# Two linked expert layers in Strassen form on one core: the order of the first pair's products, the opening's loads, the last step and GpSimd's pacing are changed

## Chip, cores and metric

The kernel runs on one core of one Trainium2 chip. The metric is the device time of one execution in microseconds (us), the median over the runs shown.

## What is computed

All inputs and the output are float32.

```python
# attention in chunks of 64 tokens: B, H, S, D = 8, 8, 576, 64
attn = softmax(q_c @ k_c.T / sqrt(D)); out = attn @ v_c
x = out as [4608, 512]
h = x @ w_in1                       # [512, 2048]
x = (max(h, 0) + alpha * min(h, 0)) @ w_out1     # [2048, 512]
h = x @ w_in2
y = (h - tanh(h)) @ w_out2          # [4608, 512]
```

## The kernel before

**Numbers.** Each float32 operand of a large product is split into a high part (a copy rounded to fp32r) and a low part (the operand less its high part). A product is then hi*hi + hi*lo + lo*hi, three matmuls.

**Supertiles and phases.** The 4608 tokens are cut into 6 supertiles of 768, and each layer goes over them once, so there are 12 supertiles, s = 0 to 11 (0 to 5 are layer 0, 6 to 11 are layer 1). Each has a phase A (the product with w_in) and a phase B (the product with w_out). Supertiles 0 and 1 do phase B in 32 plain units; from s = 2 on it is done in 28 steps of two blocks each.

**Phase A** takes the 2 x 2 blocks of x and of the weights by Strassen's scheme (Winograd's form): 8 pairs p of slices of the hidden dimension, 7 products P1 to P7 for each, so 56 products. A product is 6 matmuls of 384 columns, reads one weight block and adds into a PSUM bank. P1 and P2 share a bank, P6, P7 and P4 another, P5 and P3 a third. Between them ScalarE copies P1 to `s1` (`copy_s1`, line 925), VectorE makes u2 = s1 + bank after P6 (`sum_u2`, line 1252) and u3 = s1 + bank after P7 (`sum_u3`, line 1258). P2 waits for `s1_ready`. P7 adds into the bank that u2 is read from, and so waits for `u2_ready` (in `product`, i == 7); P4 waits for `u3_ready`. The order of the products is written out twice: as the places of their weight blocks (`product_at`) and as TensorE's calls in `phase_a` of `block.tensor`. For the first pair it is P1(0), P1(1), P5(0), P6(0), P2(0), P7(0), P6(1), P4(0); later pairs go P6, P1, P4 of the pair before, P5, P3 of the pair before, P2, P7.

**Phase B.** For each unit or step ScalarE makes the high part of g (`high_g`, line 981), VectorE the low part (`low_g`, line 1306), and TensorE waits for it (`glo_ready`). VectorE also makes Strassen's sums (`g_sum`, line 1328) and the activation (lines 1284 and 1300). In layer 1 a step's block is 9 matmuls of 256 columns over three tiles m of 128 tokens (lines 768 to 770). After the last block of the last supertile VectorE adds 768 columns to the stage (`read_y12`, line 1352) and the SyncE queue stores them (`store_quarter`, line 1610).

**Weight blocks.** A ring in SBUF holds 4 groups of 4 blocks. In supertile 0 the blocks are made in place: ScalarE writes the high part (`high_part`, 868), GpSimd the sums (`weight_sums`, 484 to 490) and the low part (`low_part`, 495). From supertile 1 on the SyncE queue loads whole groups of 1 MB from DRAM (`load_group`, 1593), three groups ahead, each when the group four before it has been used. The 168 blocks of steps and of layer 1 are made beside the other work by GpSimd, in the order of the list `MADE`: `keep_block` waits until TensorE has reached the block that `pace(k)` names, casts (510), subtracts (512) and stores 256 KB (515), with three places in turn. `pace` is a table of (supertile, count, first block, spacing in tenths of a block). `load_group` waits for the stores of the blocks in its group at s = 2 from group 14 on and at s = 6 (`made_stored`, 1592). If GpSimd falls behind the table, its blocks follow one another without pause.

**The opening.** 6 units of attention come first. SyncE's queue issues the loads of q and k, v and the raw weights in a written order. TensorE does scores (609), transposes (616) and outputs (633) of the units; VectorE subtracts the maximum and normalizes (1165 to 1189); ScalarE takes exponents (879) and copies (900, 908). Then come the splits of x (919, 1218) and its differences T1 to T4 (1214). `bank_free` holds each P1, P5 and P6 of supertile 0 until all 6 units are copied (`x_copied`).

## Time and profile before

| | us |
|---|---|
| three runs | 1540.65, 1540.56, 1536.16 |
| their median | 1540.56 |
| the profiled execution | 1540.17 |
| its span, first to last instruction | 1538.4 |
| TensorE busy in the span | 1508.9 (98%) |
| VectorE busy | 1202.3 (78%) |
| ScalarE busy | 723.7 (47%) |
| GpSimd busy | 574.3 (37%) |

The rows of the trace give a start in us from the start of the span, a duration in us, the engine (PE is TensorE, DVE is VectorE, ACT is ScalarE, POOL is GpSimd, SPq is SyncE's queue), the line of the kernel and the tiles written and read. A bracket gives the idle time of the engine before the row and what ended it. TensorE's matmuls overlap: each is issued while the one before it still runs, so what counts is the distance from start to start, and the duration of a row is longer.

### The profile page before, as it was taken

Reading aid. Unit: us, or ns where it says so; the run is one execution under the profiler, and the core shown is the slowest. Engines: PE = TensorE matmul, PEld = TensorE weight load, DVE = VectorE, ACT = ScalarE, POOL = GpSimd, SP = SyncE. Lnnn points to the kernel's source line nnn. Section 1 sums busy time; section 2 is a strip of 40 time slices with the busy share of each in tenths; the row PEclk is TensorE's granted clock in tenths of the full one; section 3 lists DMA queues with packets and bytes.
Section 4 is the critical chain, followed back from the end, with each engine's and each line's share of the span. In section 5 each row is a group of like instructions: output and inputs, shape, how many; then the busy total and the mean of one; then the engine's idle time right before and its main releaser. Section 6 shows DMA issues by size and latency. Waiting matters only on the chain.

```text
span 1538.4 us, 30313 instructions
## 1 busy us (share of the span) xinstructions
PE 1508.9 (98%) x11622; PEld 1487.0 (97%) x11622; DVE 1202.3 (78%) x1555; ACT 723.7 (47%) x1379; POOL 574.3 (37%) x756
## 2 busy tenths in 40 slices
PE   6999999999999999999999999999999999999998
PEld 5999999999999999999899999999999999999998
DVE  7998678869969987996796796786686686687684
ACT  5566465546546546652353343343344344244243
POOL 3973367877547547646736750000000000000000
PEclk8999999999999999999999999999999999999999
DMA  7795897799999899999989989768768768867765
GB/s 261 265 317 199 337 358 277 262 353 359 323 350 376 308 360 369 337 301 376 356 288 374 355 315 319 283 247 290 290 245 287 297 246 282 300 248 267 272 246 179
DMA packets 105341, 464.41 MB, mean 302 GB/s; under 512 B 12528, under 2 KB 35056, under 8 KB 62960
## 3 DMA queue, kind: packets, MB, share of 16 engines
q1 hardware_dynamic: 87344, 404.27, 73.5%
q0 software_dynamic: 17568, 57.69, 9.7%
q8 instruction: 95, 1.56, 0.4%
q10 hardware_dynamic: 288, 0.52, 0.1%
q14 instruction: 46, 0.38, 0.1%
HBM read 376.45 MB, written 85.98 MB: 301 GB/s over the span
## 4 chain that ended last, share of the span: by engine, by line
PE 84%; DVE 9%; issue 3%; DMA 2%; ACT 1%; POOL 1%; SPq 0%; DVEq 0%; ACTq 0%
PE banks L689 14%; PE banks L691 14%; PE banks L690 13%; PE banks L768 7%; PE banks L770 7%; PE banks L769 7%; PE banks L761 4%; PE banks L762 4%; PE banks L763 4%; DVE go_lo L1306 3%; PE banks L718 3%; PE banks L719 3%; PE banks L720 3%; DVE g_full L1328 2%; DVE g_full L1284 1%
## 5 line engine op out<-in xcount | busy, mean ns | idle before, releaser
L689 PE MATMUL banks<-xo_hi,ring 128*128 128x384 f32 x1344 | 454.6, 338 | 2.9 <-DMA ring<-w_split 1.4
L691 PE MATMUL banks<-xo_hi,ring 128*128 128x384 f32 x1344 | 450.2, 335 | 0.0
L690 PE MATMUL banks<-xo_lo,ring 128*128 128x384 f32 x1344 | 449.9, 335 | 0.0
L1306 DVE TENSOR_TENSOR go_lo<-g_full,go_hi 128x768 fp32r<-128x768 f32 x344 | 352.3, 1026 | 68.7 <-ACT go_hi L981 66.1
L981 ACT CAST go_hi<-g_full 128x768 fp32r<-128x768 f32 x344 | 286.1, 837 | 252.7 <-PE banks L770 101.5
L768 PE MATMUL banks<-ring,go_hi 128*128 128x256 f32 x1008 | 285.7, 283 | 0.5 <-issue 0.2
L769 PE MATMUL banks<-ring,go_hi 128*128 128x256 f32 x1008 | 285.2, 283 | 0.0
L770 PE MATMUL banks<-ring,go_lo 128*128 128x256 f32 x1008 | 285.2, 283 | 0.0
L689 PEld LDWEIGHTS banks<-xo_hi,ring 128*128 128x128 f32 x1344 | 253.0, 188 | 7.1 <-issue 2.6
L691 PEld LDWEIGHTS banks<-xo_hi,ring 128*128 128x128 f32 x1344 | 252.9, 188 | 0.4 <-issue 0.4
L690 PEld LDWEIGHTS banks<-xo_lo,ring 128*128 128x128 f32 x1344 | 253.1, 188 | 0.0
L768 PEld LDWEIGHTS banks<-ring,go_hi 128*128 128x128 f32 x1008 | 193.3, 192 | 1.0 <-issue 1.0
L769 PEld LDWEIGHTS banks<-ring,go_hi 128*128 128x128 f32 x1008 | 193.4, 192 | 0.0
L770 PEld LDWEIGHTS banks<-ring,go_lo 128*128 128x128 f32 x1008 | 193.4, 192 | 0.0
L1328 DVE TENSOR_TENSOR g_full<-g_full 128x768 f32<-128x768 f32 x160 | 166.9, 1043 | 0.0
L761 PE MATMUL banks<-go_hi,ring 128*128 128x384 f32 x448 | 150.7, 336 | 6.1 <-DVE go_lo L1306 3.1
L762 PE MATMUL banks<-go_lo,ring 128*128 128x384 f32 x448 | 149.8, 334 | 0.0
L763 PE MATMUL banks<-go_hi,ring 128*128 128x384 f32 x448 | 149.8, 334 | 0.0
L925 ACT COPY s<-banks 128x384 f32<-128x384 f32 x96 | 45.9, 479 | 173.1 <-PE banks L691 172.8
L510 POOL CAST sums<-raw 128x256 fp32r<-128x256 f32 x112 | 77.0, 687 | 132.0 <-issue 81.9
L1258 DVE TENSOR_TENSOR u<-s,banks 128x384 f32<-128x384 f32 x96 | 53.0, 552 | 91.6 <-PE banks L691 91.5
L1284 DVE SCALAR_TENSOR_TENSOR g_full<-stage,alpha_rest,g_full 128x768 f32<-128x768 f32 (+1 forms) x102 | 119.5, 1213 | 3.7 <-ACT stage L952 3.7
(138 smaller groups left out, 2346.5 us busy)
## 6 DMA issues: line engine op xcount, KB each, us to landing
ring<-w_split SPq DMA_DIRECT2D x302, 1024.0 KB, 7.1
w_split<-sums POOLq DMA_DIRECT2D x112, 256.0 KB, 6.7
w_split<-ring SPq DMA_DIRECT2D x22, 1024.0 KB, 5.5
qkv<-in_chunks SPq DMA_DIRECT2D x60, 256.0 KB, 6.9
w_split<-made_first POOLq DMA_DIRECT2D x56, 256.0 KB, 6.8
raw<-in_weights POOLq DMA_DIRECT2D x48, 256.0 KB, 7.5
x_raw<-y_between SPq DMA_DIRECT2D x6, 1536.0 KB, 10.5
out<-stage SPq DMA_DIRECT2D x24, 384.0 KB, 8.3
```

What stands on the lines that cost most here:

```text
L689: nc.tensor.matmul(h, hi, xo_hi[:, o, k, :], start=fresh and k == 0, stop=False, skip_group_check=not fresh)
L690: nc.tensor.matmul(h, hi, xo_lo[:, o, k, :], start=False, stop=False, skip_group_check=not fresh)
L691: last = nc.tensor.matmul(h, lo, xo_hi[:, o, k, :], start=False, stop=k == 1, skip_group_check=not fresh)
L761: nc.tensor.matmul(y, hi, go_hi[:, slot, e, :], start=begin, stop=False, skip_group_check=not fresh)
L762: nc.tensor.matmul(y, hi, go_lo[:, slot, e, :], start=False, stop=False, skip_group_check=not fresh)
L763: last = nc.tensor.matmul(y, lo, go_hi[:, slot, e, :], start=False, stop=end, skip_group_check=not fresh)
L768: nc.tensor.matmul(y, hi, w[:, 0, :], start=begin and m != 1, stop=False, skip_group_check=not fresh or m == 1)
L769: nc.tensor.matmul(y, hi, w[:, 1, :], start=False, stop=False, skip_group_check=not fresh or m == 1)
L770: last = nc.tensor.matmul(y, lo, w[:, 0, :], start=False, stop=end, skip_group_check=not fresh or m == 1)
L981: nc.scalar.copy(go_hi[:, go_slot(s, n), :, :], g_of(s, n)).then_inc(ghi_ready, 1)
L1306: nc.vector.tensor_tensor(go_lo[:, slot, :, :], g_of(s, n), go_hi[:, slot, :, :], ALU.subtract).then_inc(glo_ready, 1)
L1328: nc.vector.tensor_tensor(g_pairs(q, to), g_pairs(q, a), g_pairs(q, b), ALU.subtract).then_inc(t_ready, 1)
```

## The change

It has four parts. The first pair's order becomes P1(0), P1(1), P2(0), P5(0), P6(0), P7(0), in `product_at` and in TensorE's calls. In the opening the raw weights' loads move behind later loads of q, k and v, P1 and the second pair's P5 and P6 wait for 3 and 4 copied units in place of 6, and ScalarE's calls are put in another order. The last step of the last supertile does tiles 0 and 1 of both blocks first and tile 2 after them, with the sum and the store in two pieces. The table of `pace` gives 41, 17, 29, 29, 25 and 27 blocks to supertiles 1 to 6 in place of 44, 20, 27, 27, 25 and 25. The loop in `load_group` is rewritten for a group in which one of the three places has no block.

```diff
--- before.py
+++ after.py
@@ -71,7 +71,7 @@
     if i == 3:
         return base(p + 1) + 4 if p < PAIRS - 1 else 55
     if p == 0:
-        return {1: 0, 5: 2, 6: 3, 2: 4, 7: 5}[i]
+        return {1: 0, 2: 2, 5: 3, 6: 4, 7: 5}[i]
     if p == 1 and i in (1, 6):
         return 1 if i == 1 else base(1) + 1
     return base(p) + {6: 0, 1: 1, 5: 3, 2: 5, 7: 6}[i]
@@ -177,8 +177,8 @@
 
 def pace(k):
 
-    for s, count, first, tenths in ((1, 18, 2, 30), (1, 26, FIRST_BLOCKS, 12), (2, 17, 2, 26), (2, 3, 76, 110), (3, 20, 2, 26), (3, 7, 60, 70),
-                                    (4, 20, 2, 26), (4, 7, 60, 70), (5, 19, 2, 22), (5, 6, 72, 70), (6, 17, 2, 22), (6, 8, 57, 20)):
+    for s, count, first, tenths in ((1, 16, 2, 30), (1, 25, FIRST_BLOCKS, 12), (2, 15, 2, 28), (2, 2, 76, 150), (3, 21, 2, 26), (3, 8, 60, 60),
+                                    (4, 21, 2, 25), (4, 8, 60, 60), (5, 19, 2, 24), (5, 6, 72, 60), (6, 19, 2, 22), (6, 8, 57, 20)):
         if k < count:
             return s, first + tenths * k // 10
         k -= count
@@ -274,6 +274,7 @@
         ghi_ready, glo_ready = sem("ghi_ready"), sem("glo_ready")
         y_even_read, y_odd_read = sem("y_even_read"), sem("y_odd_read")
         g_first_ready, t_ready, p1_copied = sem("g_first_ready"), sem("t_ready"), sem("p1_copied")
+        last_front = sem("last_front")
         u2_copied, u3_copied = sem("u2_copied"), sem("u3_copied")
         y11_ready, y12_ready, y21_ready, y22_ready = sem("y11_ready"), sem("y12_ready"), sem("y21_ready"), sem("y22_ready")
 
@@ -640,7 +641,8 @@
                 if p >= 2:
                     pe.wait_ge({1: c11_read, 5: c12_ready, 6: c21_ready}[i], after_pairs(s, p - 2))
                 elif s == 0:
-                    pe.wait_ge(x_copied, UPS)
+
+                    pe.wait_ge(x_copied, 3 if i == 1 else 4 if p else UPS)
                 elif plain(s - 1):
                     if i == 1:
                         if p == 0:
@@ -770,6 +772,26 @@
                             last = nc.tensor.matmul(y, lo, w[:, 0, :], start=False, stop=end, skip_group_check=not fresh or m == 1)
                     last.then_inc(block_done, 1)
 
+            def last_step(s, n):
+
+                i, slot = STEPS[n][0], go_slot(s, n)
+                for e in range(2):
+                    weights_ready(s, step_at(n, e))
+                pe.wait_ge(glo_ready, go_count(s, n))
+                for tiles in ((0, 1), (2,)):
+                    for e in range(2):
+                        w = block_of(s, step_at(n, e))
+                        for m in tiles:
+                            hi, lo = go_hi[:, slot, e, m * P:(m + 1) * P], go_lo[:, slot, e, m * P:(m + 1) * P]
+                            y = banks[:, bank_pair(i) + m // 2, m % 2 * 256:(m % 2 + 1) * 256]
+                            nc.tensor.matmul(y, hi, w[:, 0, :], start=False, stop=False, skip_group_check=True)
+                            nc.tensor.matmul(y, hi, w[:, 1, :], start=False, stop=False, skip_group_check=True)
+                            last = nc.tensor.matmul(y, lo, w[:, 0, :], start=False, stop=e == 1, skip_group_check=True)
+                        if m == 2:
+                            last.then_inc(block_done, 1)
+                    if m == 1:
+                        last.then_inc(last_front, 1)
+
             def attention(s, n):
                 for u in range(UPS):
                     age = unit_age(s, u, n)
@@ -783,9 +805,9 @@
             def phase_a(s):
                 product(s, 1, 0)
                 product(s, 1, 1)
+                product(s, 2, 0)
                 product(s, 5, 0)
                 product(s, 6, 0)
-                product(s, 2, 0)
                 product(s, 7, 0)
                 product(s, 6, 1)
                 product(s, 4, 0)
@@ -824,8 +846,12 @@
                     product(s, 4, PAIRS - 1)
                     step(s, 0, (1,))
                     product(s, 3, PAIRS - 1)
-                    for n in range(1, len(STEPS)):
+                    for n in range(1, len(STEPS) - 1):
                         step(s, n)
+                    if s < RUNS - 1:
+                        step(s, len(STEPS) - 1)
+                    else:
+                        last_step(s, len(STEPS) - 1)
 
             pe.wait_ge(ident_ready, 1)
             scores(0)
@@ -1113,9 +1139,9 @@
                 nc.scalar.dma_start(here[:, 1, :], there[:, 1, :]).then_inc(qk_first_in[u], 16)
             exponent(0)
             exponent(1)
-            high_parts(0, 0)
             place_attnT(0)
             exponent(2)
+            high_parts(0, 0)
             copy_x(0)
             high_parts(0, 2)
             place_attnT(1)
@@ -1131,12 +1157,12 @@
             high_parts(0, 8)
             copy_x(3)
             high_x(0, B11)
+            place_attnT(4)
             high_x(0, B21)
-            place_attnT(4)
+            place_attnT(5)
             high_parts(0, 10)
-            place_attnT(5)
+            copy_x(4)
             high_parts(0, 11)
-            copy_x(4)
             copy_x(5)
             high_x(0, T1)
             copy_s1(0, 0)
@@ -1347,8 +1373,15 @@
 
             def read_y12(s):
 
+                dve.wait_ge(u2_copied, once(s))
+                if s == RUNS - 1:
+                    to = y_quarter(s, 0, 1)
+                    dve.wait_ge(last_front, 1)
+                    nc.vector.tensor_tensor(to[:, 0:512], to[:, 0:512], banks[:, bank_pair(3), :], ALU.add).then_inc(y12_ready, 1)
+                    dve.wait_ge(block_done, block_base(s) + blocks_of(s))
+                    nc.vector.tensor_tensor(to[:, 512:], to[:, 512:], banks[:, bank_pair(3) + 1, 0:256], ALU.add).then_inc(y12_ready, 1)
+                    return
                 dve.wait_ge(block_done, block_base(s) + blocks_of(s))
-                dve.wait_ge(u2_copied, once(s))
                 nc.vector.tensor_tensor(y_quarter(s, 0, 1), y_quarter(s, 0, 1), sum_banks(s, 3), ALU.add).then_inc(y12_ready, 1)
 
             def attention(s, n):
@@ -1587,9 +1620,9 @@
                     sp.wait_ge(w_stored[q % RING], 16 * stores_of(q))
                 if s == PLAIN and q >= 14 or s == SUPER:
                     for i in range(3):
-                        last = max(k for k in range(i, len(MADE), 3)
-                                   if MADE[k][0] == layer_of(s) and MADE[k][1] // PER_GROUP <= q)
-                        sp.wait_ge(made_stored[i], 16 * (last // 3 + 1))
+                        here = [k for k in range(i, len(MADE), 3) if MADE[k][0] == layer_of(s) and MADE[k][1] // PER_GROUP <= q]
+                        if here:
+                            sp.wait_ge(made_stored[i], 16 * (here[-1] // 3 + 1))
                 sp.dma_start(ring[:, group % RING, :, :, :].rearrange("x b h n -> x (b h n)").bitcast(F32),
                              w_dram[dram_group(layer_of(s), q, plain(s)), :, :]).then_inc(ring_in[group % RING], 16)
 
@@ -1673,12 +1706,12 @@
             load_first_qk(0)
             load_first_qk(1)
             load_first_v(0)
-            load_raw(0)
             load_first_qk(2)
             load_first_v(1)
-            load_raw(1)
+            load_raw(0)
             load_first_qk(3)
             load_first_v(2)
+            load_raw(1)
             load_first_qk(4)
             load_first_v(3)
             load_first_qk(5)
@@ -1692,9 +1725,13 @@
                     make_groups(s)
                 else:
                     load_groups(s)
-            store_quarter(RUNS - 1, 0, 1)
+            for count, tiles in ((0, 2), (1, 1)):
+                sp.wait_ge(y12_ready, once(RUNS - 1) + count)
+                here = stage[:, 2 * HALF + 512 * count:2 * HALF + 512 * count + 256 * tiles]
+                sp.dma_start(out_tiles[SUPER - 1, 3 + 2 * count:3 + 2 * count + tiles, :, 0:256].rearrange("j p d -> p j d"),
+                             here.rearrange("x (j d) -> x j d", j=tiles)).then_inc(y_stored[0], 16)
             for half in range(2):
-                sp.wait_ge(y_stored[half], 16 * y_stores(RUNS - 1))
+                sp.wait_ge(y_stored[half], 16 * (y_stores(RUNS - 1) + (half == 0)))
             for i in range(RING):
                 sp.wait_ge(w_stored[i], 16 * sum(1 for g in range(i, group_base(1), RING)))
```

## Rows read from the trace of the kernel before

**Rows 1.** First line of the page.

```profile
span 1538.4 us, 30313 instructions
```

**Rows 2.** Engines' busy time by stretch: start of phase B, s = 2; phases B, s = 5, 7.

```profile
378.00:398.00 20.00, 18.27 (x101) 17.18 (x101) 19.60 (x20) 8.69 (x12) 17.58 (x22) 1.00 0.94 314
...
757.00:820.00 63.00, 60.61 (x349) 60.03 (x348) 60.87 (x61) 31.40 (x40) 32.28 (x40) 1.00 0.88 300
...
996.00:1058.00 62.00, 62.00 (x513) 62.00 (x512) 51.83 (x59) 31.63 (x41) 0.00 (x0) 1.00 0.72 257
```

**Rows 3.** Timeline of TensorE, s = 9: last matmul of P6(0), first of P7(0).

```profile
1181.69 0.33 PE L691 MATMUL banks<-xo_hi,ring 128*128 128x384 f32 x1
...
1182.91 0.34 PE L689 MATMUL banks<-xo_hi,ring 128*128 128x384 f32 x1
```

**Rows 4.** Timelines of VectorE and ScalarE, s = 9: u2 of pair 0, copy of P1(0).

```profile
1182.12 0.55 DVE L1252 TENSOR_TENSOR u<-s,banks 128x384 f32<-128x384 f32 x1 [3.27 <-PE banks L691]
...
1178.94 0.48 ACT L925 COPY s<-banks 128x384 f32<-128x384 f32 x1 [6.63 <-PE banks L691]
```

**Rows 5.** Timelines where TensorE waited for VectorE, s = 2, step 2.

```profile
384.38 1.15 DVE L1306 TENSOR_TENSOR go_lo<-g_full,go_hi 128x768 fp32r<-128x768 f32 x1
...
385.67 0.41 PE L761 MATMUL banks<-go_hi,ring 128*128 128x384 f32 x1 [0.74 <-DVE go_lo L1306]
385.92 0.34 PE L762 MATMUL banks<-go_lo,ring 128*128 128x384 f32 x1
```

**Rows 6.** Timeline of the opening and of the first products.

```profile
2.13 1.07 SPq L1570 DMA_DIRECT2D raw<-in_weights  x2
...
10.32 1.05 DVE L1189 TENSOR_TENSOR probs<-probs,row_inv 128x512 f32<-128x512 f32 x1
...
10.65 1.14 PE L609 MATMUL banks<-g_full 64*64 64x64 f32 x32 [3.72 <-DMA g_full<-in_chunks]
...
11.85 0.69 DVE L1165 TENSOR_REDUCE row_max<-banks 128x8 f32<-128x512 f32 x1 [0.48 <-PE banks L609]
...
31.30 0.58 ACT L908 COPY x_raw<-banks 128x512 f32<-128x512 f32 x1 [0.35 <-PE banks L633]
...
31.98 0.66 PE L689 MATMUL banks<-xo_hi,ring 128*128 128x384 f32 x1 [0.75 <-issue]
...
38.69 0.54 DVE L1252 TENSOR_TENSOR u<-s,banks 128x384 f32<-128x384 f32 x1
...
39.33 0.41 PE L689 MATMUL banks<-xo_hi,ring 128*128 128x384 f32 x1
```

**Rows 7.** Timeline of the end: VectorE's last sum.

```profile
1534.40 0.95 DVE L1352 TENSOR_TENSOR stage<-stage,banks 128x768 f32<-128x768 f32 x1 [4.59 <-PE banks L770]
```

**Rows 8.** Timeline of GpSimd, s = 2: its first idle time.

```profile
405.80 4.15 POOL L510 CAST sums<-raw 128x256 fp32r<-128x256 f32 x1 [7.36 <-issue]
```

**Rows 9.** Groups of VectorE by line, s = 2: 384 to 398, then 404 to 441 us.

```profile
L1306 DVE TENSOR_TENSOR go_lo<-g_full,go_hi 128x768 fp32r<-128x768 f32 x6 | 8.1, 1358 | 0.0
...
L1306 DVE TENSOR_TENSOR go_lo<-g_full,go_hi 128x768 fp32r<-128x768 f32 x17 | 16.8, 986 | 2.2 <-ACT go_hi L981 2.0
```

**Rows 10.** Timelines of GpSimd's stores, SyncE's ring loads and TensorE in s = 6.

```profile
866.17 0.56 POOL L515 DMA_DIRECT2D w_split<-sums  x1 [0.30 <-POOL sums L512]
...
873.01 0.56 POOL L515 DMA_DIRECT2D w_split<-made_first  x1 [0.30 <-POOL made_first L512]
...
875.44 0.80 SPq L1593 DMA_DIRECT2D ring<-w_split  x2
...
882.66 0.28 PE L768 MATMUL banks<-ring,go_hi 128*128 128x256 f32 x1
...
913.36 0.56 POOL L515 DMA_DIRECT2D w_split<-sums  x1 [0.30 <-POOL sums L512]
...
918.88 0.80 SPq L1593 DMA_DIRECT2D ring<-w_split  x2
```

**Rows 11.** DMA issues, 875.0 to 875.8 us: count, KB, us to landing.

```profile
ring<-w_split SPq DMA_DIRECT2D x1, 1024.0 KB, 4.8
```

## Prediction

> **What bounds the kernel now.** I read the busy times first, then TensorE's row of starts block by block, and at each gap the row of the engine that ended it. TensorE is the bound nearly everywhere. In phase B of s = 7 it is busy 62.00 of 62.00 us, and the same holds from s = 7 to the end; only earlier is there something to save: 1.73 us idle in the first 20 us of phase B of s = 2, 2.39 us in phase B of s = 5 [rows 2]. There VectorE is the one that is late (19.60 of 20 us and 60.87 of 63 us busy), while GpSimd works beside it. So the reader should ask of each part: does it put a wait into a stream of matmuls that has none, and which of the few early waits does it take out?
>
> **P2 third.** No product is added or removed. What moves is the cover between P6(0) and P7(0). P7(0) adds into the bank that u2 is made from, so it needs P6(0) finished, then VectorE's sum, then the signal. Before, P2(0) ran in that time. At s = 9 the last matmul of P6(0) starts at 1181.69 and P7(0) at 1182.91: seven starts later, so one start is (1182.91 - 1181.69) / 7 = 0.174 us, and six of these are P2(0) [rows 3]. VectorE's sum starts at 1182.12 and takes 0.55, so it ends 0.98 us after P6(0)'s last start [rows 4]. From such an end to TensorE's first matmul: 384.38 + 1.15 = 385.53, and the matmul starts at 385.67, 0.14 us later [rows 5]. The chain is 0.98 + 0.14 = 1.12 us and the cover was 1.22 us: hidden, by 0.1 us. After the change P7(0) comes right behind P6(0); the cover is 0.174 us, and 1.12 - 0.17 = 0.95 us is a wait. The matmul that starts after a wait holds its successor back too: 385.92 - 385.67 = 0.25 us in place of 0.174 [rows 5], 0.07 us more. Each first pair costs **1.0 us**. The bounds are 0.9 (signal 0.1 us, no hold) and 1.05.
>
> What does P2 third give back? P2(0) needs the copy of P1(0), which ends at 1178.94 + 0.48 = 1179.42 [rows 4]; it would start twelve starts ahead of 1181.69 + 0.17, at 1179.78, so it doesn't wait, but with only 0.3 us to spare. P5(0) and P6(0) come one product later, and in supertiles 1 to 11 they had no wait to lose. Behind the waiting P7(0) stand P6(1), P4(0) and the rest of TensorE's queue; VectorE's u3 waits for P7(0) and moves with it. VectorE had stood idle 3.27 us before u2 [rows 4], so it can't use the 1.0 us to catch up either; its later work hangs on products that are late by as much. I therefore count all of supertiles 1 to 11: 11 x 1.0 = **+11.0 us** (9.9 to 11.5).
>
> In supertile 0 the wait is there already: u2 starts at 38.69, after VectorE's splits of x, and P7(0) at 39.33 [rows 6]. No charge there.
>
> **The opening.** Unit 2's scores start at 10.65, on the load of q and k; VectorE goes on at 11.85, after 0.48 us of idle time [rows 6]. The load now takes the place of two raw loads that held the queue from 2.13 for 1.07 us, so it is issued 1.1 us sooner. VectorE can then go on when its normalization ends, 10.32 + 1.05 = 11.37: 0.48 us gained. That normalization ran beside GpSimd's weight sums, which now start later; it might be shorter, but the same GpSimd work then meets a later normalization. From 11.85 to unit 5's output VectorE and the units follow one another, so the gain arrives. P1(0) starts at 31.98, after the copy of unit 5, 31.30 + 0.58 [rows 6]; it no longer waits for it, 0.7 us sooner. But u2 and P7(0) hang on T1 to T3, which still need that copy, so what lasts is the shift of the copy. I take **-0.7** (nothing to -1.5). A raw load now lands later, and the casts behind it on ScalarE stand ahead of unit 1's copy: up to 0.3 us back, inside this range.
>
> **The last step.** The last sum takes 0.95 us for 768 columns [rows 7]; 384 columns take 0.55 [rows 4], so 256 take about 0.95 - 512 x (0.40 / 384) = 0.42: -0.53 us. The first piece, about 0.7 us long, can start six matmuls before the end and just fits. The second store is a third as large, and the first is still in flight in the same queue: nothing to -0.5. I take **-0.6** (-0.3 to -1.0). TensorE does the same 18 matmuls. The rewritten loop in the ring's loads names the same stores: nothing.
>
> **GpSimd's table.** Through s = 1 and 2 GpSimd is behind its table (in s = 2 by over 20 us), so it works without pause, and only the number of its blocks counts, some 3.4 us each ((873.01 - 866.17) / 2 [rows 10]). Before, the run is 43 blocks long and ends at 398.4, where its first idle time begins (405.80 - 7.36 [rows 8]); now it has 40 from the same start, so it ends three blocks, 10 us, sooner, near 388. In 384 to 398 us VectorE's low parts take 1.36 us on average, in 404 to 441 us 0.99 [rows 9]: nine such operations and more get 0.4 us shorter. The idle time at 385.67 stays, most of what follows it goes: **-1.6** of some 2.6 us (0 to -2.6). The Trainium skill (SBUF — State Buffer, section "Who interferes with whom") says that VectorE and GpSimd share a port pair as an exclusive lock, the loser blocked for the other's whole instruction. By that rule even more is freed here, the full -2.6, and the sum below would be 1550; the rows show an operation stretched by 0.4 us on average, and I go by them. The blocks taken out here reappear: one more in phase A and one in phase B of s = 3 and 4, two more in s = 6. I charge +0.5, +0.3 and +0.4 us of VectorE's waits (0 to 1 us each).
>
> **The ring in s = 6.** Here the change meets a limit. GpSimd is behind its table in s = 6 as well, and group 15 of the ring needs made block 154. That was stored from 866.17, and SyncE's queue could issue only at 875.44, though TensorE had left the ring's place 12 blocks of 1.04 us before 882.66, at 870.2 [rows 10]. The load took 4.8 us [rows 11], so it landed at 880.3; TensorE needs the group at 882.66 [rows 10]: 2.4 us to spare. Now two blocks stand ahead, and block 154 is stored where block 156 was, at 873.01 [rows 10]: 6.8 us later. TensorE is 1.0 us later. If the store takes as long as before (9.3 us to the queue's release) the group lands at 882.3 + 4.8 = 887.1, 3.4 us late; if it takes the 5.5 us of the last block (913.36 to 918.88 [rows 10]) it lands at 883.4 and is just in time. The second is nearer, as the DMA queues are idle while SyncE waits. The last made block is the same case again: issued 913.36 + 7, released at 926, landed at 931, needed near 929 with the delays. Together **+1.5** (0 to +6).
>
> **Sum.** Against the profiled execution, 1540.17 us (a span of 1538.4 [rows 1] and 1.8 us around it), 0.4 us below the median of the runs: +11.0 - 0.7 - 0.6 - 1.6 + 0.5 + 0.3 + 0.4 + 1.5 = +10.8, so 1551.0 us.
>
> **Rivals.**
> 1. **The late ring decides** in s = 6: both groups at their upper bound, +6 and more in place of +1.5. 1540.2 + 15.3 = 1555.5 or above. For it: the queue already waited 5 us there twice. Against: the store is fast when nothing else loads. 0.12.
> 2. **The waits are absorbed** in supertiles 1 to 6, where TensorE waits later for VectorE anyway: 1.0 us there is worth nothing. Left are 5 x 1.0 in s = 7 to 11 and the rest of the sum: 1545. Against: VectorE is idle before u2. 0.10.
> 3. **Faster:** the early waits all go. From s = 1 to s = 6 TensorE's waits for VectorE and for loads come to some 12.8 us; if fewer blocks of GpSimd, and a pause of TensorE in which the engines and queues ahead catch up, remove them all, the sum is +11.0 - 0.7 - 0.6 - 12.8 = -3.1, 1537 us. It decides from 9.7 us removed. Against: s = 3, 4 and 6 get more blocks, not fewer. 0.04.
> 4. **No wait at P7(0):** only if P7 did not need u2; `product` says it does. That the change doesn't do what it says I give 0.01, near 1538.5.
>
> The forecast has 0.73. What a measurement of this kernel can tell is about 0.3%, 4.6 us: slower means above 1545.2. The forecast and the first rival are slower, the second lies on the line. Faster 0.04, same 0.08, slower 0.88. The forecast's own range is 1547 to 1554; with half of the first two rivals, 1545.5 to 1556.5.
>
> **What would show it.** At each first P7 of s = 1 to 11 TensorE's row should show a wait of 0.9 us, released by VectorE's line of u2, also in s = 7 to 11, where TensorE is now never idle. GpSimd's run in s = 2 should end 10 us earlier, and the gaps behind step 4 be gone. SyncE's queue should stand before groups 15 and 25 in s = 6. I am wrong if P7(0) starts 0.17 us behind P6(0), or if the later gaps of s = 2 to 6 shrink by what the first pairs lose.

## The result and the profile after

The changed kernel takes 1547.83 us (median of 5 runs, 1546.71 to 1550.94), beside 1540.56 for the kernel before (5 runs, 1536.16 to 1542.66). The two medians lie 7.3 us apart. The ratio on record, with its 95% interval, is 1.0057 [1.0042, 1.0073], which is 8.8 us, between 6.5 and 11.2: slower, clear of noise. The forecast was 1551.0, with a range from 1545.5 to 1556.5. The profiled execution took 1546.71 us.

The first place to look is TensorE's row where P7(0) follows P6(0). The next three fences are timelines of the kernel after at s = 9: TensorE, VectorE, and ScalarE with the copy of P1(0). They answer to [rows 3] and [rows 4].

```profile
1187.30 0.34 PE L693 MATMUL banks<-xo_hi,ring 128*128 128x384 f32 x1
1188.39 0.41 PE L691 MATMUL banks<-xo_hi,ring 128*128 128x384 f32 x1 [0.75 <-issue]
1188.64 0.34 PE L692 MATMUL banks<-xo_lo,ring 128*128 128x384 f32 x1
```

```profile
1187.73 0.55 DVE L1278 TENSOR_TENSOR u<-s,banks 128x384 f32<-128x384 f32 x1 [4.24 <-PE banks L693]
```

```profile
1183.51 0.48 ACT L951 COPY s<-banks 128x384 f32<-128x384 f32 x1 [6.63 <-PE banks L693]
```

The last matmul of P6(0) starts at 1187.30 and P7(0) at 1188.39, 1.09 us later, where one start takes 0.174. That is 0.916 us of waiting. (The bracket says 0.75, since it counts from the end of the matmul before.) The next matmul comes 0.25 us after it, another 0.075. So the first pair loses 0.99 us, and it does so in each of s = 1 to 11. VectorE's u2 ends at 1187.73 + 0.55 = 1188.28, and P7 starts 0.11 us behind it. The copy of P1(0) ends at 1183.51 + 0.48 = 1183.99, and P2(0) starts at 1184.35 without a wait: 0.36 us to spare, as reckoned.

In the list of what TensorE waited for, in the kernel after, these waits stand under "issue" and not under VectorE (columns: us in all, times, longest). They are the first line here. The second line is P7(0) of supertile 0. Before, the same line of the kernel had one wait under "issue", that of P1(0) of supertile 0, and none at any P7(0) of s = 1 to 11.

```profile
PE banks L691 <- issue: 8.2, 11, 0.8
...
PE banks L691 <- DVE u L1278: 1.4, 1, 1.4
```

The reader should not stop at the word "issue": it is what the profile writes where it saw no releaser at the moment of the start. Here the sum had ended 0.11 us earlier, and only the two timelines side by side show the cause.

The busy time by stretch of the kernel after answers to [rows 2]: the first 20 us of phase B of s = 2, and then phases B of s = 3 to 7.

```profile
378.00:398.00 20.00, 20.00 (x118) 20.00 (x117) 18.80 (x25) 10.47 (x14) 3.09 (x6) 1.00 0.88 315
506.30:570.00 63.70, 61.11 (x350) 60.21 (x349) 61.78 (x62) 31.81 (x42) 34.20 (x41) 1.00 0.93 333
637.80:702.00 64.20, 61.47 (x349) 60.05 (x349) 62.82 (x62) 32.14 (x42) 32.78 (x40) 1.00 0.91 310
759.20:822.00 62.80, 61.56 (x349) 60.05 (x349) 59.80 (x62) 32.15 (x42) 29.23 (x35) 1.00 0.87 313
879.20:942.60 63.40, 62.89 (x518) 62.69 (x518) 59.17 (x59) 31.79 (x41) 31.85 (x39) 1.00 0.88 328
999.80:1062.40 62.60, 62.60 (x518) 62.60 (x518) 51.82 (x59) 31.43 (x40) 0.00 (x0) 1.00 0.73 258
```

In s = 2 TensorE has no idle time left in these 20 us; GpSimd works 3.09 us there in place of 17.58. In s = 3 and 4 GpSimd's column has grown, and VectorE's with it. The same two phases in the kernel before:

```profile
508.50:570.90 62.40, 61.06 (x351) 60.34 (x350) 58.72 (x61) 31.85 (x41) 26.99 (x34) 1.00 0.91 328
637.50:698.80 61.30, 60.79 (x349) 60.21 (x349) 59.14 (x62) 32.56 (x42) 24.96 (x32) 1.00 0.89 307
```

At s = 4 GpSimd goes from 32 to 40 instructions and VectorE from 59.14 of 61.30 us to 62.82 of 64.20. What TensorE waited for in that stretch was one wait of 0.4 us before, and after it is this:

```profile
PE banks L763 <- DVE go_lo L1332: 1.5, 2, 1.3
PE banks L763 <- issue: 1.2, 1, 1.2
```

In phase B of s = 3 TensorE's longest wait is not for VectorE but for a weight group of the ring. The kernel before has none there:

```profile
PE banks L763 <- DMA ring<-w_split: 1.0, 1, 1.0
```

I cut each span at the starts of the stages' first matmuls. The last two columns are means over the profiled executions of the kernels of this study with the old table and without the wait (five), and with the new table and the wait (three):

| us | before | after | mean, old table, no wait | mean, new table, wait |
|---|---|---|---|---|
| up to phase B of s = 0 | 92.83 | 92.28 | | |
| phases A, s = 1 to 6 | 383.30 | 385.67 | 383.87 | 386.20 |
| phases B, s = 2 to 6 | 314.14 | 314.67 | 312.74 | 315.36 |
| phases A, s = 7 to 11 | 280.89 | 285.80 | 280.91 | 285.77 |
| last matmul's start to the end | 4.29 | 3.31 | | |

Phases A of s = 7 to 11 pay the full price, 4.9 us for five waits. Phases A of s = 1 to 6 pay 2.4 us for six (2.3 by the means). The opening and the tail give 0.55 and 0.98 us back, phase B of s = 0 takes 0.32, and with phases B of s = 2 to 6 it makes the span's 1544.9 - 1538.4 = 6.5 us.

The opening in the kernel after, in answer to [rows 6]: unit 2's scores, the normalization, GpSimd's first sum of weights, VectorE going on, the first product, the copy of unit 5.

```profile
8.21 1.13 PE L610 MATMUL banks<-g_full 64*64 64x64 f32 x32 [1.38 <-DMA g_full<-in_chunks]
...
9.76 0.69 DVE L1215 TENSOR_TENSOR probs<-probs,row_inv 128x512 f32<-128x512 f32 x1
...
10.27 0.76 POOL L485 TENSOR_TENSOR sums<-raw 128x256 f32<-128x256 f32 x1 [8.80 <-DMA raw<-in_weights]
...
10.37 0.68 DVE L1191 TENSOR_REDUCE row_max<-banks 128x8 f32<-128x512 f32 x1
...
30.62 0.69 PE L691 MATMUL banks<-xo_hi,ring 128*128 128x384 f32 x1
...
30.75 0.59 ACT L934 COPY x_raw<-banks 128x512 f32<-128x512 f32 x1
```

VectorE goes on at 10.37 in place of 11.85. The load is earlier, so there is no idle time, and the normalization takes 0.69 in place of 1.05 us: GpSimd's first sum now starts at 10.27, near its end, and no longer stands beside all of it. Of these 1.48 us the copy of unit 5 keeps 0.55.

The end in the kernel after, in answer to [rows 7]:

```profile
1541.28 0.69 DVE L1380 TENSOR_TENSOR stage<-stage,banks 128x512 f32<-128x512 f32 x1 [3.95 <-PE banks L789]
...
1541.61 0.28 PE L789 MATMUL banks<-ring,go_lo 128*128 128x256 f32 x1
...
1541.92 0.42 DVE L1382 TENSOR_TENSOR stage<-stage,banks 128x256 f32<-128x256 f32 x1
```

The first piece of the sum runs under the last matmuls, and the second takes 0.42 us as reckoned. The last store of the output landed 2.1 us after its issue in place of 2.6.

The ring in s = 6, in answer to [rows 10]: the stored block that group 15 needs, and SyncE's load; then TensorE's first matmul on the group, and its first on group 16. Ahead of them, GpSimd's first pause in s = 2, in answer to [rows 8].

```profile
402.27 1.01 POOL L511 CAST sums<-raw 128x256 fp32r<-128x256 f32 x1 [20.80 <-issue]
...
872.91 0.56 POOL L516 DMA_DIRECT2D w_split<-sums  x1 [0.30 <-POOL sums L513]
...
879.96 6.25 SPq L1626 DMA_DIRECT2D ring<-w_split  x4
...
885.70 0.28 PE L770 MATMUL banks<-ring,go_hi 128*128 128x256 f32 x1
...
890.69 0.39 PE L770 MATMUL banks<-ring,go_hi 128*128 128x256 f32 x1 [0.51 <-DMA ring<-w_split]
```

```profile
ring<-w_split SPq DMA_DIRECT2D x1, 1024.0 KB, 5.2
```

Block 154 is stored from 872.91, 0.1 us from the forecast's 873.01. The load of 5.2 us lands at 885.2 and TensorE takes it at 885.70, without a wait: 0.5 us to spare. The next load was held up in the queue too: it was issued 0.5 us behind the first, took 10.2 us and landed at 890.6, and there TensorE waited 0.51 us. In the second profile of the changed kernel that load took 9.4 us and landed 0.4 us ahead of its use. Group 25 landed at 927.9, 1.7 us ahead of its use.

### The profile page after: what moved, and what is told of

Read it like the earlier page. It is cut to its first block, busy times and chain, and to the rows that moved or that the text cites. A ratio compares the mean times of both kernels' runs of the same rounds, so it can differ in the third digit from the quotient of the medians.

```text
span 1544.9 us, 30314 instructions
## 1 busy us (share of the span) xinstructions
PE 1510.2 (98%) x11622; PEld 1485.0 (96%) x11622; DVE 1208.1 (78%) x1556; ACT 723.8 (47%) x1379; POOL 566.1 (37%) x756
## 4 chain that ended last, share of the span: by engine, by line
PE 87%; DVE 6%; issue 3%; DMA 2%; POOL 1%; ACT 1%; SPq 0%; DVEq 0%; ACTq 0%; POOLq 0%
PE banks L691 14%; PE banks L692 14%; PE banks L693 14%; PE banks L770 8%; PE banks L772 8%; PE banks L771 8%; PE banks L763 4%; PE banks L764 4%; PE banks L765 4%; PE banks L720 3%; PE banks L721 3%; PE banks L722 3%; DVE go_lo L1332 2%; DMA ring<-w_split 1%; DVE g_full L1310 1%
## 5 line engine op out<-in xcount | busy, mean ns | idle before, releaser
L513 POOL TENSOR_TENSOR sums<-raw,sums 128x256 fp32r<-128x256 f32 x112 | 116.0, 1036 | 9.2
```

## The experiments

Eleven runs on three chips. Each median stands beside that of the kernel before on the same chip (1539.92, 1539.48 and 1539.50), except the first, which is a single execution. Where two kernels ran on different chips, their ratios to the kernel before are the better comparison. All were profiled once. The diffs show the lines that carry each edit, and `...` stands for what is left out.

**The kernel before, once more.**

> The kernel before, unchanged, profiled once more, to see how much TensorE's waits vary between two executions. If the waits before late loads (1.95 us before an output of unit 16 in s = 1, 1.58 us in the middle of phase A of s = 5) belong to the order of the work, both stand again within 0.5 us; if they are chance of the DMA queues, one or both are gone. The waits for VectorE in s = 2 to 6 should stand again within 0.3 us each. P7(0) has no wait in s = 1 to 11 by either theory.

1537.52 us, span 1535.7. TensorE's waits for loads in phase A of s = 1 differ between the two executions of the same kernel. Before, and then again:

```profile
PE a_bank L633 <- DMA qkv<-in_chunks: 1.6, 2, 1.0
```

```profile
PE a_bank L633 <- DMA qkv<-in_chunks: 1.1, 1, 1.1
```

Phase B of s = 5 took 63.25 and 61.41 us, so the waits for VectorE there did not stand again within the 0.3 us that was expected. One profile carries about 2 us of such chance, so stages are compared by means over several kernels below.

**P2 third alone.** The new order on the kernel before, and the rewritten loop of `load_group`, which names the same stores. Everything else is old.

```diff
-        return {1: 0, 5: 2, 6: 3, 2: 4, 7: 5}[i]
+        return {1: 0, 2: 2, 5: 3, 6: 4, 7: 5}[i]
...
+                product(s, 2, 0)
                 product(s, 5, 0)
                 product(s, 6, 0)
-                product(s, 2, 0)
                 product(s, 7, 0)
```

> The kernel before with P2 of the first pair third, and nothing else. Theory (the cover between P6(0) and P7(0) is gone): TensorE waits 0.91 us at P7(0) in each of s = 1 to 11, each supertile loses 0.99 us, 10.9 us in all, 1551 us; the other waits stay. Rival (waits are absorbed by later ones where VectorE is late): 0.99 us in s = 7 to 11 alone, 5 us in all, and the waits of s = 2 to 6 in phase B shrink by as much. Rival (the slowdown is the ring's or the table's): no more than 1 us slower.

1549.58 against 1539.92: 1.0058 [1.0044, 1.0072], +9.7 us by the medians, 6.8 to 11.1 by the interval. TensorE's waits:

```profile
PE banks L689 <- issue: 9.0, 12, 0.8
```

This one edit costs all that the whole change costs. Eleven of the twelve waits are P7(0) of s = 1 to 11; the twelfth is P1(0) of s = 0, which the kernel before has too. P7(0) of s = 0 waits as well, filed under GpSimd. There the fourth product starts 0.8 us later than before, and that is the granted clock: from 36 to 38 us it is 0.55 of full speed here, near the lower level of 1.2 GHz, and 0.98 in the kernel before (second line).

```profile
36.00:38.00 2.00, 2.00 (x8) 2.00 (x8) 2.00 (x3) 1.47 (x3) 1.38 (x2) 0.55 0.01 4
```

```profile
36.00:38.00 2.00, 2.00 (x13) 2.00 (x12) 2.00 (x3) 1.47 (x3) 1.44 (x2) 0.98 0.01 4
```

**P2 back in the fifth place, the rest of the change kept.**

```diff
-        return {1: 0, 2: 2, 5: 3, 6: 4, 7: 5}[i]
+        return {1: 0, 5: 2, 6: 3, 2: 4, 7: 5}[i]
...
-                product(s, 2, 0)
                 product(s, 5, 0)
                 product(s, 6, 0)
+                product(s, 2, 0)
                 product(s, 7, 0)
```

> The changed kernel with the old order of the first pair (P1, P1, P5, P6, P2, P7). Theory: 10.9 us faster than the changed kernel in s = 1 to 11, up to 1 us given back in the opening, as P5(0) again needs T1 as the third product: 1537 to 1538 us, faster than before by 3 to 4 us. Rival (table and ring cause the slowdown): 1546 us or more, no faster than the changed kernel.

1539.38: 0.9997 [0.9987, 1.0008]. Against the changed kernel that is 8.4 us less, and against the kernel before nothing: the 3 to 4 us that were expected below it are not there.

**P2 third, but P5 and P6 exchanged,** so that P5(0) stands between P6(0) and P7(0).

```diff
-        return {1: 0, 2: 2, 5: 3, 6: 4, 7: 5}[i]
+        return {1: 0, 2: 2, 6: 3, 5: 4, 7: 5}[i]
...
                 product(s, 2, 0)
-                product(s, 5, 0)
                 product(s, 6, 0)
+                product(s, 5, 0)
                 product(s, 7, 0)
```

> The changed kernel with P5(0) and P6(0) exchanged, so that P5(0) runs while VectorE makes u2: P1, P1, P2, P6, P5, P7. The work is the same. Theory (only the missing cover costs): the 0.91 us wait at P7(0) is gone in s = 1 to 11 though P2 is still third, 10.9 us less than the changed kernel, 1537 us, 0.2% below before. Rival (P2 third costs in another way, by the place of its block in the ring or the earlier copy of P1): the time stays near 1547 us. If P6(0) now waits for T2 in the opening, that wait is there in place of the one at P7(0), and P7(0) starts when it did.

1539.81: 0.9999 [0.9988, 1.0010], 8.0 us less than the changed kernel, though not the 1537 that was expected. TensorE and then VectorE at s = 9; the first row is the end of P6(0), the second the last matmul of P5(0), the third P7(0):

```profile
1180.48 0.33 PE L693 MATMUL banks<-xo_hi,ring 128*128 128x384 f32 x1
...
1181.52 0.34 PE L693 MATMUL banks<-xo_hi,ring 128*128 128x384 f32 x1
1181.70 0.34 PE L691 MATMUL banks<-xo_hi,ring 128*128 128x384 f32 x1
```

```profile
1180.91 0.56 DVE L1278 TENSOR_TENSOR u<-s,banks 128x384 f32<-128x384 f32 x1 [3.20 <-PE banks L693]
```

u2 ends at 1181.47 and P7 starts at 1181.70, 0.174 behind the matmul ahead of it. P2 is third here too. So its early place costs nothing by itself; what costs is that nothing stands between P6 and P7.

**The new table alone.**

```diff
-    for s, count, first, tenths in ((1, 18, 2, 30), (1, 26, FIRST_BLOCKS, 12), (2, 17, 2, 26), (2, 3, 76, 110), (3, 20, 2, 26), (3, 7, 60, 70),
+    for s, count, first, tenths in ((1, 16, 2, 30), (1, 25, FIRST_BLOCKS, 12), (2, 15, 2, 28), (2, 2, 76, 150), (3, 21, 2, 26), (3, 8, 60, 60),
...
```

> The kernel before with the new table of GpSimd's blocks, and nothing else. From the profile of the changed kernel: TensorE's idle time in phase B of s = 2 falls by 2.5 to 3 us, in s = 3 and 4 it rises by 1.4 and 2 to 3 us, s = 6 doesn't change; no difference in sum, 1539 to 1542 us. Rival: the rise in s = 3 and 4 came from the shifted first pair, and the table alone saves 3 us, 1537 us. SyncE's queue stands before groups 15 and 25 of s = 6 longer than before, but TensorE waits there under 1 us.

1540.98 against 1539.48: 1.0007 [0.9997, 1.0018]. Its phases B of s = 2 and s = 4:

```profile
378.40:438.90 60.50, 60.50 (x350) 60.33 (x349) 54.62 (x62) 32.54 (x42) 9.04 (x12) 1.00 0.89 318
...
637.80:701.00 63.20, 61.46 (x349) 60.11 (x348) 61.63 (x61) 31.79 (x41) 30.47 (x37) 1.00 0.91 308
```

The waits of s = 2 are all gone, 2.9 us less than the 63.39 of the kernel before. But s = 4 takes 63.25 in place of 61.35. Means of six kernels with each table, phases B of s = 2 to 6: 63.00, 62.35, 61.34, 62.76, 63.29 with the old one, and 60.69, 63.25, 63.56, 64.26, 63.82 with the new one. That is -2.3, +0.9, +2.2, +1.5 and +0.5, together +2.8 us. Two things stand beside these means. In s = 3 five of the six kernels with the new table wait 0.3 to 1.0 us for a group of the ring near 553 us, and none with the old one does. In s = 4 the changed kernel takes 64.25 and 64.21 in its two profiles and the other four 63.21 to 63.25, and why it takes 1 us more is open.

**The opening alone.**

```diff
-            load_raw(0)
             load_first_qk(2)
             load_first_v(1)
-            load_raw(1)
+            load_raw(0)
...
```

> The kernel before with the opening's loads, ScalarE's order and the shorter waits of P1, P5 and P6 in supertile 0 alone; P2 stays fifth. Forecast of the text: VectorE's chain to unit 5 is 0.5 to 1.3 us shorter, and phase B of supertile 0 starts 0.5 us earlier or more, since P7(0) hangs on VectorE's splits of x. If P2 third had its own part in that, phase B starts no earlier than before (92.8 us in the first profile, 93.2 in the second).

1539.50: 1.0002 [0.9990, 1.0013]. Phase B of s = 0 begins at 92.58 in place of 92.83 and 93.19: 0.25 to 0.6 us earlier, where 0.5 or more was expected. Its phase A of s = 2 takes 71.61 in place of 66.94, with waits for loads that the kernel before doesn't have there:

```profile
PE a_bank L633 <- DMA qkv<-in_chunks: 1.9, 2, 1.3
PE a_bank L609 <- DMA qkv<-in_chunks: 0.9, 2, 0.5
```

The last two of these waits, 0.61 and 1.32 us, stand 2 us apart at 372.4 and 374.4, and behind them the granted clock falls to 0.50, the lower level of 1.2 GHz:

```profile
376.00:378.00 2.00, 2.00 (x8) 2.00 (x7) 0.35 (x1) 1.98 (x4) 1.62 (x4) 0.50 0.47 178
```

From 374.3 to 376 it is 0.58, so 1 to 1.7 us of the 4.7 is an estimate for the clock. In no other profile does a phase after that of s = 0 show a granted clock below 1.00.

**The last step alone.**

```diff
-            store_quarter(RUNS - 1, 0, 1)
+            for count, tiles in ((0, 2), (1, 1)):
+                sp.wait_ge(y12_ready, once(RUNS - 1) + count)
```

> The kernel before with the last step by tiles alone. From TensorE's last matmul to the end of the span it was 4.29 us in both profiles of before; expected 3.3 us, as in the changed kernel: the last sum 0.5 us shorter and the rest in the store. No other stage changes; the time is 1 us less, too little for the runs to tell.

1538.65: 0.9993 [0.9983, 1.0002]. From the last matmul's start to the end it takes 3.31 us, against 4.29 or 4.30 in every kernel with the old end: -0.98.

**P5 and P6 exchanged, with the old table.** The version above with P5 as cover, less the new table.

```diff
-    for s, count, first, tenths in ((1, 16, 2, 30), (1, 25, FIRST_BLOCKS, 12), (2, 15, 2, 28), (2, 2, 76, 150), (3, 21, 2, 26), (3, 8, 60, 60),
+    for s, count, first, tenths in ((1, 18, 2, 30), (1, 26, FIRST_BLOCKS, 12), (2, 17, 2, 26), (2, 3, 76, 110), (3, 20, 2, 26), (3, 7, 60, 70),
...
```

> The changed kernel with P5(0) and P6(0) exchanged and the old table of GpSimd's blocks. If the new table gives back in s = 3 to 5 what it saves in s = 2, TensorE's idle time in phases B of s = 2 to 6 is 8 to 11 us, against 11 to 12.5 us with the new table, and the time 1 us below the exchange with the new table: 1538.5 us. Rival: the new table is worth 2 us or more, and this is slower than the exchange with the new table by that.

1537.30: 0.9985 [0.9976, 0.9994], the lowest median of all, about 2 us below the kernel before (0.9 to 3.7 by the interval). Against the same kernel with the new table it is 2.5 us less by the medians and 2.2 by the ratios. Its phase B of s = 4 is back at the old length:

```profile
635.70:697.00 61.30, 60.79 (x349) 60.21 (x349) 58.93 (x61) 32.19 (x42) 24.51 (x32) 1.00 0.89 305
```

**The cover moved one product on.** P6(1) stands between P6(0) and P7(0), so that P4(0) comes right behind P7(0).

```diff
                 product(s, 6, 0)
-                product(s, 7, 0)
                 product(s, 6, 1)
+                product(s, 7, 0)
                 product(s, 4, 0)
```

> The changed kernel with P6(1) moved ahead of P7(0): P1, P1, P2, P5, P6(0), P6(1), P7(0), P4(0). P6(1) now covers u2, but nothing stands between P7(0) and P4(0), which needs u3. Theory (each of VectorE's sums needs one product of cover, 1.04 us): no wait at P7(0), 0.9 us of wait at P4(0) in s = 1 to 11, and the time of the changed kernel, 1548 us. Rival (it is P2's place that costs): P2 is still third, so the time is the same but the wait stays at P7(0) or is spread.

1549.76: 1.0064 [1.0049, 1.0079]. TensorE at s = 9: the end of P6(1), the first and last matmul of P7(0), the first of P4(0). Then VectorE's u3.

```profile
1191.36 0.34 PE L693 MATMUL banks<-xo_hi,ring 128*128 128x384 f32 x1
1191.53 0.34 PE L691 MATMUL banks<-xo_hi,ring 128*128 128x384 f32 x1
...
1192.40 0.34 PE L693 MATMUL banks<-xo_hi,ring 128*128 128x384 f32 x1
1193.43 0.41 PE L691 MATMUL banks<-xo_hi,ring 128*128 128x384 f32 x1 [0.69 <-issue]
```

```profile
1192.78 0.55 DVE L1284 TENSOR_TENSOR u<-s,banks 128x384 f32<-128x384 f32 x1 [1.48 <-PE banks L693]
```

P7(0) no longer waits and P4(0) waits instead, 1193.43 - 1192.40 - 0.17 = 0.86 us, for u3, which ends at 1193.33. The price belongs to two products on one bank that follow one another with a sum between them, and not to P7 or u2.

**The changed kernel once more.**

> The changed kernel once more, profiled again. The 0.91 us at each P7(0) and the idle times of phases B in s = 2 to 6 (0.3, 3.5, 4.1, 2.6, 0.8 us) should stand again within 1 us each; waits for late loads in phases A may come and go, up to 2 us in a place. 1548 us.

1547.15: 1.0050 [1.0035, 1.0066]. The wait at P7(0) is the same to 0.01 us in all of s = 1 to 11. The idle time stands again within 1 us in four of the five phases B but not in s = 5, which takes 64.51 in place of 62.84.

**A third table,** on the kernel with P5 as cover: s = 1 as in the change, one block more in s = 2, and blocks of s = 3 to 5 moved from phase A and the start of phase B to late in phase B.

```diff
+    for s, count, first, tenths in ((1, 16, 2, 30), (1, 25, FIRST_BLOCKS, 12), (2, 15, 2, 28), (2, 3, 76, 110), (3, 19, 2, 26), (3, 9, 70, 45),
+                                    (4, 19, 2, 26), (4, 9, 70, 45), (5, 18, 2, 24), (5, 8, 72, 45), (6, 19, 2, 22), (6, 8, 57, 20)):
...
```

> P5(0) and P6(0) exchanged, and a table of GpSimd's blocks of my own: as in the changed kernel for s = 1 and 2 but for one block more, 19 and 9 in s = 3 and 4, where the 9 begin at block 70 and not at 60, 18 and 8 in s = 5. If TensorE's waits at steps 2 and 4 come from GpSimd's blocks that run into phase B beside VectorE, they shrink in s = 3 and 4 from 1.5 to 2.7 us to under 0.5 us each; the blocks moved later cost 0.3 us each where they meet VectorE. Sum in phases B 7 us against 11 to 12: 1535 to 1537 us, the fastest version. Rival (only the number of GpSimd's blocks in a phase B counts): no better than the exchange with the old table, 1537.3 us.

1541.40: 1.0011 [1.0000, 1.0021], 1.6 us above the same kernel with the new table, where 1535 to 1537 was expected. Phases B of s = 3 and 4:

```profile
505.20:568.80 63.60, 61.69 (x349) 59.86 (x348) 61.83 (x62) 32.41 (x42) 29.04 (x34) 1.00 0.91 327
635.50:699.20 63.70, 61.74 (x349) 59.79 (x348) 62.18 (x62) 32.55 (x42) 29.75 (x36) 1.00 0.88 303
```

The waits leave the early steps and come back in late ones. And in s = 6 the ring is late:

```profile
PE banks L770 <- DMA ring<-w_split: 1.2, 1, 1.2
```

So pushing the blocks late gained nothing here. Their number alone doesn't decide either: in s = 3 GpSimd has 34 instructions here as under the old table, and the phase takes 63.65 in place of 62.35. What would place them best stays open.

## Why the prediction was right, and where two errors met

**The wait at P7(0)** was right in mechanism, place and size: 1.0 us forecast, 0.99 measured (0.916 and 0.075 in place of 0.95 and 0.07). The signal took 0.11 us in place of 0.14. That VectorE can't catch up there was right too. The forecast looked for it under VectorE's line of u2; the profile files it under "issue".

**"I therefore count all of supertiles 1 to 11"** is the step that failed: 11 x 1.0 is the sum of the waits and not their price. In s = 7 to 11, where nothing else is waited for, they cost 4.9 us. In phases A of s = 1 to 6 the six cost 2.3 us with the old table (386.21 in one profile, less the mean of 383.87) and 3.1 by the means with the new one (386.20 - 383.15), where six times 0.99 are 5.9. The phase of 71.61 us in "the opening alone" lifts the first mean by 1 us; without that profile the price is 3.4. So it is about half of the full one. The single stages tell why. Phase A of s = 1 takes 67.99 to 68.23 in the four kernels that wait, and anything from 66.97 to 69.02 in the nine that don't; s = 5 takes 57.15 to 57.27 and 56.17 to 57.87. The shortest of those without the wait, plus 1.0, is what those with it take, to within 0.3 us. All other waits of TensorE in phases A of s = 1 to 6 come to 2.5 us in the mean of the nine kernels without this wait (1.2 to 4.9) and to 0.4 in the four with it (0 to 1.1). So the wait is added in full to the best case, and takes away about 2 us of waits that come and go. That TensorE's pause gives late loads the time to land is the reading that fits; no run tests it by itself. The second rival, in which all six are absorbed, was half right, and the third, in which the early waits all go, fell. By the medians, P2 third costs 9.7 us alone, 8.4 and 8.0 in the whole change (with P2 back, and with P5 as cover). The term should have been about +8 to +9, not +11.0. The interval of the run with P2 third alone doesn't exclude 11 by itself; the stages do.

**Supertile 0** was costed at nothing, because "the wait is there already". The wait was 0.17 us before and is 1.58 in the changed kernel. But VectorE's u2, which stands behind its splits of x, sets the start of P7(0) both times, and P7(0) starts at 38.79 in place of 39.33: the longer wait costs nothing. With P2 third alone phase B of s = 0 begins at 93.92, 0.7 to 1.1 later than in the four profiles with the old opening and order. About 0.8 us of that is the low granted clock from 36 to 38 us in this one execution, so it is not shown that the order costs anything there.

**The opening** was sized at -0.7. The four profiles with the old opening and order begin phase B of s = 0 at 92.8 to 93.2, mean 93.0, the eight with the new opening at 91.6 to 92.6, mean 92.2: about -0.85.

**The tail** was sized at -0.6 and is -0.98: the sum gave the 0.53, and the last store's landing 0.48, close to the upper bound of 0.5 that the forecast gave it.

**GpSimd's table** was mis-sized and with the wrong sign: -1.6 + 0.5 + 0.3 + 0.4 = -0.4 forecast, +2.8 by the means of phases B. In s = 2 it was better than forecast, -2.3 by the means. The forecast kept the wait at 385.67 and took out what follows it; that wait went too. GpSimd's run ended at 402.27 - 20.80 = 381.5, ahead of this place, and not near 388, as its blocks took (381.5 - 245.2) / 40 = 3.4 us each in place of (398.4 - 246.3) / 43 = 3.5, beside being three fewer. The Trainium skill (SBUF — State Buffer, section "Who interferes with whom") calls the shared port pair an exclusive lock, and by it the forecast named -2.6; the measured -2.3 lies nearer to that than to my -1.6. That doesn't bear the rule out: the run of blocks ended 7 us earlier than either reckoning assumed. What was missed are the other supertiles. The forecast put one more block into phase B of s = 3 and 4, at 0.5 and 0.3 us. The windows show 7 and 8 more of GpSimd's instructions there, of some three for each block, and the phases take 0.9 and 2.2 us longer. VectorE had 2.2 us idle in 61.3 at s = 4, and a forecast should have asked how much of that was left. The late group of the ring in s = 3 is another part. In s = 5 the forecast charged nothing, the number of blocks is the same, and the phase takes 1.5 us longer by the means; why is open. By whole runs the table costs 1.5 us alone (the interval of its ratio reaches from -0.5 to +2.8) and 2.5 between the two kernels with P5 as cover (1539.81 and 1537.30). In phases A no difference shows: 383.87 and 383.15 by the means, 382.8 and 383.15 without the profile that has the phase of 71.61 us.

**The ring in s = 6**, +1.5, was a middle between in time and late. Group 15 was in time by 0.5 us, and group 16, on which the forecast put nothing, was late by 0.5 in one profile and not in the other. The first rival fell; with the third table the wait at group 16 is 1.2 us. Block 154 was stored when forecast, but by luck: all of s = 6 began 2.1 us later than before, and TensorE reached the group 3.0 us later, where the forecast took 1.0. The store held the queue for 7.0 us, between the 5.5 and 9.3 of the forecast. The queues were not idle meanwhile, as the forecast has it: before, the DMA engines were 0.65 busy from 870.8 to 875.4.

**The sum** with measured terms, the means beside those of the old table: +4.9 + 2.3 - 0.85 - 0.98 + 2.8 = +8.2 us, and +9.3 if the six waits are taken at 3.4. The medians show +7.3, the ratio +8.8 and the span of the one profile +6.5. The forecast's +10.8 had P2 too dear by 2 to 4, the ring too dear by at least 1 and the table too cheap by 3. So the forecast came within 3.2 us of the result partly because its errors had opposite signs; the mechanism that decides the verdict was right.

## What to carry to other kernels

When an order of products is rewritten, look for each pair that shares an accumulator with another engine's read between them, and keep at least one whole product between the two. Here that makes seven starts, 1.22 us, against a chain of 1.09 from the last matmul's start to the next one. P2, P5 and P6(1) all served. A wait that is certain costs its full length only where its engine waits for nothing else: here it was paid in full in the stages that are 100% busy, and by about half in those that already had waits. Work of GpSimd that is moved beside a nearly full VectorE (59 of 61 us) is not free at the place where it lands, even if the place that it leaves gets better.

## What the runs showed of the hardware

VectorE starts to read a bank 0.43 us after the start of the last matmul into it (1187.30 to 1187.73), its sum of 384 columns takes 0.55 us, and TensorE starts 0.11 us after it ends. With the 0.075 us that the first matmul holds the next one back, such a handover costs 1.0 us if nothing covers it, and is the same to 0.01 us in 33 places of three executions (1.086 to 1.090 us from start to start). The two executions of the same kernel differ by 2.6 us (1540.17 and 1537.52), and the trace puts nearly all of it into phases B of s = 2 to 6 (314.14 and 311.73), with waits for loads in phases A that come and go. In one profile of thirteen two such waits of 0.61 and 1.32 us, 2 us apart, were followed by a granted clock of 0.50 for some 2 us.
